# Attention and two expert layers on one core: moving operands of small matrix products made wider

## The reference, cut to what matters

```python
# attention: B, H, S, D = 4, 8, 768, 48
for t in range(S):
    kt, vt, rt = k[:, :, t], v[:, :, t], r[:, :, t]
    cur = einsum('bhd,bhe->bhde', u * kt, vt)
    y[:, :, t] = einsum('bhd,bhde->bhe', rt, state + cur)
    state = w * state + einsum('bhd,bhe->bhde', kt, vt)
x = y as (3072 tokens, 384)
# layer 1: E = 8 experts, each takes cap = 384 tokens
logits = x @ w_gate                     # (3072, 8)
for idx in argsort(-logits.flatten()):  # greedy: best pair first
    tok, e = idx // E, idx % E
    if token taken or expert full: continue
    assign tok to e
out[mask_e] = relu(x[mask_e] @ w1[e]) @ w2[e]
# layer 2: all 8 experts for every token, weighted by P
P = exp(logits2 - max); 8 rounds of row and column normalization
out = sum_e P[:, e] * (relu(x @ w1[e]) @ w2[e])
```

## Time and profile before

| | us |
|---|---|
| median of three runs | 2113.72 |
| profiled execution, whole | 2112.88 |
| its span, first to last instruction | 2111.2 |
| TensorE busy with products | 2049.4 (97%) |
| TensorE weight loads (beside products) | 1877.4 (89%) |
| VectorE, ScalarE, GpSimd busy | 842.6, 520.4, 361.9 |
| mean granted clock of TensorE | 0.974 |

### The profile page before, as it was taken

One profiled execution on the slowest core, in us unless ns is written; L12 is line 12 of the kernel. 1 busy time (PEld: TensorE's weight loads), 2 busy tenths in 40 slices (PEclk: granted clock), 3 DMA queues, 4 the chain that ended last, 5 costly groups with the idle time before them and its releaser, 6 DMA issues.

```text
span 2111.2 us, 31403 instructions
## 1 busy us (share of the span) xinstructions
PE 2049.4 (97%) x12372; PEld 1877.4 (89%) x12372; DVE 842.6 (40%) x1710; ACT 520.4 (25%) x915; POOL 361.9 (17%) x395
## 2 busy tenths in 40 slices
PE   8984999999999999999999999999999999999998
PEld 7983888899989999899998999989999899998997
DVE  7767777852532323223232232322323223232232
ACT  4540322244221311222122122121311122122121
POOL 8732111265000300030011003000300030012101
PEclk9985988999999999999999999999999999999999
DMA  7721222333000100010001000000100010000000
GB/s 275 238 92 72 100 75 76 110 139 124 1 1 0 60 0 0 0 60 0 0 6 53 0 0 30 30 0 0 60 0 0 0 60 0 0 0 15 27 17 30
DMA packets 18687, 92.33 MB, mean 44 GB/s; under 512 B 2880, under 2 KB 6080, under 8 KB 14528
## 3 DMA queue, kind: packets, MB, share of 16 engines
q1 hardware_dynamic: 13248, 56.85, 7.6%
q0 software_dynamic: 5376, 34.61, 4.5%
HBM read 82.01 MB, written 9.44 MB: 43 GB/s over the span
## 4 chain that ended last, share of the span: by engine, by line
PE 87%; DVE 4%; issue 1%; POOL 1%; DMA 1%; ACT 0%; DVEq 0%; POOLq 0%
PE bank L705 83%; PE bank L802 2%; PE bank L752 1%; PE bank L822 1%; DMA x_in<-x_dram,home 1%; DVE reached L1171 0%; DVE w_lo L1099 0%; DVE slot L1068 0%; POOL x_in L1420 0%; PE bank L808 0%; DVE w_lo L1104 0%; PE bank L745 0%; DVE choice L165 0%; DVE best L145 0%; DVE moved L1189 0%
## 5 line engine op out<-in xcount | busy, mean ns | idle before, releaser
L705 PE MATMUL bank<-x_hi,w_hi 128*128 128x512 f32 (+1 forms) x1344 | 522.2, 389 | 3.0 <-DVE h_lo L1053 3.0
L705 PE MATMUL bank<-x_hi,w_lo 128*128 128x512 f32 (+1 forms) x1344 | 516.2, 384 | 0.0
L705 PE MATMUL bank<-x_lo,w_hi 128*128 128x512 f32 (+1 forms) x1344 | 516.2, 384 | 0.0
L705 PE MATMUL bank<-w_hi,h_hi 128*128 128x384 f32 x1536 | 514.0, 335 | 0.0
L705 PE MATMUL bank<-w_hi,h_lo 128*128 128x384 f32 x1536 | 513.7, 334 | 0.0
L705 PE MATMUL bank<-w_lo,h_hi 128*128 128x384 f32 x1536 | 513.4, 334 | 0.0
L986 ACT ACTIVATE h_hi<-bank 128x512 fp32r<-128x512 f32 x384 | 229.6, 598 | 1128.6 <-PE bank L705 1128.6
L1378 DVE SCALAR_TENSOR_TENSOR h_lo<-bank,h_hi 128x512 fp32r<-128x512 f32 x384 | 265.8, 692 | 547.2 <-ACT h_hi L986 547.2
L705 PEld LDWEIGHTS bank<-x_hi,w_hi 128*128 128x128 f32 x1344 | 254.5, 189 | 48.4 <-issue 3.3
L705 PEld LDWEIGHTS bank<-x_hi,w_lo 128*128 128x128 f32 x1344 | 254.4, 189 | 45.1
L705 PEld LDWEIGHTS bank<-x_lo,w_hi 128*128 128x128 f32 x1344 | 254.5, 189 | 44.0
(11 more groups left out here) (187 smaller groups left out, 1544.4 us busy)
## 6 DMA issues: line engine op xcount, KB each, us to landing
w_raw<-moe_w_dram SPq DMA_DIRECT2D x16, 1536.0 KB, 6.6
rows_in<-rkv_rows_dram SPq DMA_DIRECT2D x24, 576.0 KB, 5.0
rkT<-rk_turned_dram SPq DMA_DIRECT2D x24, 512.0 KB, 3.9
x_dram<-x_rows SPq DMA_DIRECT2D x24, 192.0 KB, 5.0
x_in<-x_dram,home POOLq DMA_INDIRECT x24, 3.3
out_dram<-sums,home POOLq DMA_INDIRECT x24, 2.5
w_raw<-moe_w_dram,w_row POOLq DMA_INDIRECT x16, 7.3
u_tok<-u_rows_dram SPq DMA_DIRECT2D x1, 192.0 KB, 5.0
```

The costliest lines, as they stand in the source:

```text
L705: done = nc.tensor.matmul(out_tile, a, b, start=first and n == 0, stop=last and n == len(terms) - 1, skip_group_check=True)
```

## The change

- The product of the scores with v for one head gets a moving operand of 96 columns: v of that head twice. The second copy goes to 48 columns of bank 4 beside y, the same ones for every head.
- The gate of layer 1 has its weights padded with ones to 128 columns, the second gate to 96. The added results fall on columns that are written later or not read.
- A count reads its choice four times (32 columns), homes read their operand 16 times (96 columns). Only the first copy is read. The places in banks 3, 4 and 7 are moved accordingly.
- TensorE, as soon as the first three constants are there, forms 16 products of ones with 512 columns in bank 7, then two before and two after the scores of tile 0, four before and two after those of tile 1.
- POOL fills the padding of both gates (two memsets more, counted in `CONSTS`), and the two loads of the gates go to 8 of the columns of each row.

Nothing is removed, and no other order or wait is changed.

```diff
     PLACE_PARTS = 4
+    COUNT_COPIES = 4
+    HOME_COPIES = 16
+    WIDE = 96
     SLOTS = 6
...
         before_bf = sb(whole, "before_bf", [P, P], BF16)
-        gate2 = sb(whole, "gate2", [P, DT, E])
+        gate2 = sb(whole, "gate2", [P, DT, WIDE])
         w1_raw = sb(whole, "w1_raw", [P, DT, F])
...
             x_rows = sb(early, "x_rows", [P, T, DM])
-            gate1 = sb(early, "gate1", [P, DT, E])
+            gate1 = sb(early, "gate1", [P, DT, P])
 
...
                 xT_ps = banks[6][:, 0:DM]
-                logit_ps = banks[7][:, 0:T * E]
+                logit_ps = banks[7]
                 table_ps = banks[6]
...
                 same_set, logits_ahead = sem(ctx, "same_set"), sem(ctx, "logits_ahead")
-                CONSTS = 8
+                CONSTS = 10
 
...
                         load_tile(2)
-                        sp.dma_start(gate1[:], moe_w_gate).then_inc(gates_loaded, 16)
-                        sp.dma_start(gate2[:], moe2_w_gate).then_inc(gates_loaded, 16)
+                        sp.dma_start(gate1[:, :, 0:E], moe_w_gate).then_inc(gates_loaded, 16)
+                        sp.dma_start(gate2[:, :, 0:E], moe2_w_gate).then_inc(gates_loaded, 16)
                         for t in range(3, SLOTS):
...
                         nc.gpsimd.memset(k_tok[:, :, :, D:HW], 0.0).then_inc(const_ready, 1)
+                        nc.gpsimd.memset(gate1[:, :, E:P], 1.0).then_inc(const_ready, 1)
+                        nc.gpsimd.memset(gate2[:, :, E:WIDE], 1.0).then_inc(const_ready, 1)
                         pool.wait_ge(const_ready, CONSTS)
...
 
+                        def with_spare(h):
+                            partitions = y_ps.ap[0]
+                            return bass.AP(y_ps.tensor, y_ps.offset + h * D, [partitions, [DM - h * D, 2], [1, D]])
+
                         def y_of(t):
...
                                 for h in (2 * q, 2 * q + 1):
-                                    last = nc.tensor.matmul(y_ps[:, h * D:(h + 1) * D], scores[:, t % 2, h % 2, q],
-                                                            rows_in[:, t % SLOTS, 2, h * D:(h + 1) * D],
+                                    last = nc.tensor.matmul(with_spare(h), scores[:, t % 2, h % 2, q],
+                                                            rows_in[:, t % SLOTS, 2, h * D:(h + 1) * D].unsqueeze(1).to_broadcast([P, 2, D]),
                                                             start=(c == 0), stop=True, skip_group_check=True)
...
                             for d in range(DT):
-                                last = nc.tensor.matmul(logit_ps[:, t * E:(t + 1) * E], xT[:, t % 2, d], gate1[:, d],
+                                last = nc.tensor.matmul(logit_ps[:, t * E:t * E + P], xT[:, t % 2, d], gate1[:, d],
                                                         start=(d == 0), stop=(d == DT - 1), skip_group_check=True)
 
+                        def keep_busy(n):
+                            for _ in range(n):
+                                nc.tensor.matmul(banks[7][:].rearrange("p (a b) -> p a b", b=P), ones_bf[:],
+                                                 ones_bf[:].unsqueeze(1).to_broadcast([P, 4, P]), start=True, stop=True,
+                                                 skip_group_check=True)
+
+                        pe.wait_ge(const_ready, 3)
+                        keep_busy(16)
                         pe.wait_ge(const_ready, CONSTS)
                         for t in range(T):
+                            if t < 2:
+                                keep_busy(2 + 2 * t)
                             scores_of(t)
+                            if t < 2:
+                                keep_busy(2)
                             if t == 2:
...
             H_BANKS = 3
-            count_ps, moved_ps, tally_ps = banks[3][0:NJ, 0:E], banks[3][:, E:2 * E], banks[3][:, 2 * E:3 * E]
-            logits2_ps = banks[4][:, CAP:CAP + CT * E]
+            moved_ps, tally_ps = banks[3][:, 0:E], banks[3][:, E:2 * E]
+            count_ps, count_wide = banks[3][0:NJ, P:P + E], banks[3][0:NJ, P:P + COUNT_COPIES * E]
+            logits2_ps, logits2_wide = banks[4][:, CAP:CAP + CT * E], banks[4][:, CAP:]
             ties_ps = banks[7][:, 0:1]
             ranks_ps = banks[7][:, 4:6]
-            home_ps = banks[7][:, 8:8 + 2 * CT]
+            home_ps, home_wide = banks[7][:, 8:8 + 2 * CT], banks[7][:, 8:8 + HOME_COPIES * 2 * CT]
 
...
                         for d in range(DT):
-                            last = nc.tensor.matmul(logits2_ps[:, j * E:(j + 1) * E],
+                            last = nc.tensor.matmul(logits2_wide[:, j * E:j * E + WIDE],
                                                     x2T[:, d, CAP * s + j * P:CAP * s + (j + 1) * P], gate2[:, d],
...
                                 pe.wait_ge(reached_ready, 2 * n + 2 * t // T + 1)
-                            last = nc.tensor.matmul(count_ps, reached[:, t], choice[:, :, t],
+                            last = nc.tensor.matmul(count_wide.rearrange("p (c n) -> p c n", c=COUNT_COPIES), reached[:, t],
+                                                    choice[:, :, t].unsqueeze(1).to_broadcast([P, COUNT_COPIES, E]),
                                                     start=(t == 0), stop=(t == T - 1))
...
                                 pe.wait_ge(places_ready, PLACE_PARTS * c + PLACE_PARTS * t // T + 1)
-                            last = nc.tensor.matmul(home_ps, is_place[:, :, t], token_at[:, :, :, t].rearrange("p a s -> p (a s)"),
+                            tokens = token_at[:, :, :, t].rearrange("p a s -> p (a s)")
+                            last = nc.tensor.matmul(home_wide.rearrange("p (c n) -> p c n", c=HOME_COPIES), is_place[:, :, t],
+                                                    tokens.unsqueeze(1).to_broadcast([P, HOME_COPIES, 2 * CT]),
                                                     start=(t == 0), stop=(t == T - 1))
```

## The result

The changed kernel takes 2172.04 us (2170.51 to 2173.24) against 2114.38 of the kernel before, a ratio of 1.0275 with a 95% interval of 1.0263 to 1.0288: 58 us more where 13.5 less were forecast. One of the four runs of the kernel before, 2200.01 us, was in the slower state that some executions fall into, and the ratio leaves it out. Its profiled execution took 2171.88 us, the span is 2170.1.

What follows compares the result with a forecast made beforehand. TensorE, busy 97% of the span, was taken as the bound. Gains of 1.8, 3.2, 1.0 and 9.6 us, less 1.8 for gates and 0.3 for later ends, made 13.5: from 2112.9 to 2099 us, range 2090 to 2111.

Steps and rivals of the forecast that it cites:

- The counts: Counts in the 56 searches: 32 columns hidden under the instruction start, cost 0; 7.7 us if loads and products didn't overlap.
- The homes: Homes in the search: 96 columns cost 0 at 71 ns a product; 7.8 us if the widening came on top.
- The dips: Clock dips in the search phases, beginning as the homes end: gone with wider homes, gain 9.6 us.
- Ahead of the third phase: First expert products, 207 to 216.56 us: wider counts may lift the clock sooner, gain 1.0 us, ends 0 and 3.1.
- The end of attention: Last y block, turn and gate: wider products keep the clock up, gain 3.2 us; end nothing.
- Gates at 128 columns: First gates in attention, 6 a tile: widening costs 1.8 us, ends 0 and 3.6.
- y at 96 columns: y products in attention, 16 a tile in 24 tiles: widening costs 0, load spacing staying at 112 ns.
- The start: First two scores: products of ones raise the clock early, gain 1.8 us, ends 2.5 and nothing.
- The small packets: Gate loads ahead of tiles 3 to 5: 512 more packets, at most 4.3 us delay, taken as 0.
- Within phases 0 and 1: First two search phases: wider counts would not keep the clock up, and it wouldn't matter much.
- (a): Search: homes still don't hold the clock, in part or whole; gain 3.9 us, 2109 us; chance 0.17.
- (d): Every widened product: columns not hidden behind loads, 52 us less the clock's 16, 2149 us; chance 0.05.

Runs made afterwards that it cites:

- e1: The changed kernel with the counts back at 8 columns, all else as changed; 2129.54 us, ratio 1.0079 to the kernel before.
- e4: The changed kernel, all widths kept, with choice and token operands stored so that moving columns lie 2 bytes apart; 2101.64 us, ratio 0.9947.
- e3: The changed kernel with counts back at 8 columns and homes back at 6; 2105.92 us, ratio 0.9963 to the kernel before.
- e6: The kernel of e4 (columns 2 bytes apart) with counts at 8 columns and homes at 6; 2109.67 us, ratio 0.9978.
- e9: The kernel of e4 run again unchanged on a third chip, as the measure for those beside it; 2107.61 us, ratio 0.9969.
- e10: The kernel of e9 with the first gate back at 8 columns; 2105.39 us, ratio 0.9955 to the kernel before.
- e12: The kernel of e9 without the products of ones, memsets and widths kept; 2109.39 us, ratio 0.9978 to the kernel before.

## Why the prediction was wrong, step by step

**The counts: the step that failed first.** The prediction took 32 columns as "27 ns at the lower level (0.32 / 384 = 0.83 ns a column) and 14 at the full one. So 0". The 0.83 was read from products whose columns lie side by side. The count's columns lie 24 bf16 apart, as the slice [:, :, t] says, and such a column takes 1.8 ns at either clock. Measured +0.80 us a count, 56 x 0.80 = 45 us by the durations and 42.5 us by e1. Even the bound of the prediction for products without overlap, 7.7 us in the cold counts, was far below. The price of the distance between columns was missing from the sum, and the counts' term stood at 0.

**The homes failed in the same way.** "With 96 columns homes stream 43 of the 71 ns" was 174 ns for one. Measured 20.2 us (8 x 2.37 = 19 by the durations), where the upper bound was 7.8. The 8-column and 6-column rows could not show it: 15 and 11 ns lie under floors of 27 and 71.

**The dips.** "I expect the dips gone: gain 9.6" failed in the changed kernel: each of its phases holds one. In e4 they were gone. Its four phases take 163.1 us in the profiled execution, those of e3 170.9, so 7.8 us less where the prediction had 8.3 for them; the whole executions differ by as much, 2102.25 and 2109.98. The medians differ by 4.3 only, 2101.64 and 2105.92, since most executions of e3 kept the clock up for longer than the profiled one. But e6 kept it with narrow homes, so that the width of the homes did this is not shown, and the mechanism of the prediction stays open here.

**Ahead of the third phase** the forecast was 1.0, ends 0 and 3.1. In the changed kernel the clock rose 4.4 us after the first expert product where it was 9.1, an estimated 2.3 us.

**The end of attention** was right: forecast 3.2. From the last y block to the first count it is 8.64 us (142.36 to 151.00) where it was 12.19 (141.63 to 153.82), 3.55 less. **Gates at 128 columns**, forecast +1.8 us: some 2 between e9 and e10, and unnecessary. **y at 96 columns**, 0: 113 ns, right. **The start**, forecast 1.8: the third scores come 2.0 us earlier in the profiled execution, but right behind them TensorE waits 0.91 us for VectorE's state where it waited 0.37, so 1.4 are left. e12 finds at most 0.35 of it to be due to the products of ones in its own execution. **The small packets** of the gates delayed nothing that shows. **Within phases 0 and 1** the clock stayed at 0.50, as taken.

**A reading.** The slices with a clock below full in the earlier trace rows are the third, fourth, sixth and seventh, not the third to the tenth. No term rests on it.

**The rivals.** (a), that the homes don't hold the clock, came true in the changed kernel. (d), slower at 2149, had the right place in part and the wrong mechanism: it charged all widened products alike, and the rule of the Trainium skill that it leaned on ("TensorE: Matmul & The Clock Gate", Part 3), that a load doesn't overlap a product of the same rows, does not hold here: y at 96 columns costs nothing. The costs that (d) gave to y and gates, 26 us, are about 2 where they were measured; those it gave to counts and homes, 27, are 64. The parts make up the time: 2112.9, less the 8 of e3, and 45 + 19 for counts and homes by their durations are 2169, where 2172 was measured.

## What to carry to other kernels

Spare columns exist where a weight load or an issue floor sets the spacing, but ask how far apart the columns of the moving operand lie before you price them: steps of 16 and 48 bytes between bf16 columns cost 1.8 ns a column, four times the 0.45 of adjacent ones at the full clock, and a narrow product hides it under its floor. Wider operands with adjacent columns cost nothing in counts and homes and went with an earlier rise of the clock (counts) and with a later fall (y, or the gates). Where two widenings each suffice, take the cheaper: y at 96 columns without gates at 128 gave the best ratio of its chip, 0.9955.

## What the runs showed of the hardware that was not expected

- A bf16 moving operand read in steps of 48 bytes takes 1.8 ns a column, independent of the granted clock: 59 ns for 32 columns at both levels. In steps of 16 bytes 96 columns took about as long (24 products in 4.51 us against 4.38). Steps of 2 and 4 bytes show no such cost.
- Such slow products did not hold the clock: in homes of 4.07 us in which TensorE was busy throughout, it fell from 1.00 to 0.50 between 243 and 244 us.
- The same kernel took 40.6 us from homes to homes on one chip and 41.3 to 41.5 on another, both at clock 1.00 (e4 and e9).
- Padding two tensors that the expert layers don't read went with products 2% slower there (5996 against 6112 in 1200 us on one chip). The cause is open.
